# Gated scan and ELU feed-forward: activation and ring rows a little more than a row apart, and the first product read and written backwards

## What is computed

```
sig = 1.0 / (1.0 + np.exp(-f_logit))
f = lower_bound + (1.0 - lower_bound) * sig
for t in range(S):                      # 6080 steps
    h = f[:, t] * h + (1.0 - f[:, t]) * x[:, t]
    y[:, t] = h
h = y.reshape(12160, 256) @ w_in        # 256 -> 2048
g = np.where(h > 0.0, h, np.exp(np.minimum(h, 0.0)) - 1.0)
out = g @ w_out                         # 2048 -> 256
```

## Time and profile before

| | before |
|---|---|
| median of two runs | 989.77 us (989.63 and 989.91) |
| span of the profiled execution | 987.9 us |
| PE busy | 983.2 us, 4362 matmuls |
| PE weight loads busy | 817.7 us |
| ACT, DVE, POOL busy | 791.6, 726.4, 633.2 us |
| chain that ended last | PE 100% |
| granted TensorE clock | 1.000 |

### The profile page before, as it was taken

How to read it: one execution, slowest core, us unless ns; L and a number is a source line. 1 busy time by engine, 2 the same in 40 slices (tenths; PEclk the granted TensorE clock), 3 DMA queues, 4 the chain that set the end, 5 groups by cost and what they waited for, 6 DMA issues and landing times.

```text
span 987.9 us, 15016 instructions
## 1 busy us (share of the span) xinstructions
PE 983.2 (100%) x4362; PEld 817.7 (83%) x4362; DVE 726.4 (74%) x916; ACT 791.6 (80%) x1424; POOL 633.2 (64%) x477
## 2 busy tenths in 40 slices
PE   9999999999999999999999999999999999999998
PEld 6998888888888888888888888888888888888887
DVE  6987876976886796697688679678768867956444
ACT  7988878878888887877887887888788788787775
POOL 2588796576567558557656756856765765675444
PEclk9999999999999999999999999999999999999999
DMA  7212012002102201200210210120021021001001
GB/s 265 66 33 91 0 35 63 33 1 76 54 1 60 69 1 42 64 21 10 65 53 0 64 63 0 51 66 10 25 61 42 0 74 53 0 0 45 1 1 43
DMA packets 23078, 42.02 MB, mean 43 GB/s; under 512 B 2560, under 2 KB 4096, under 8 KB 23040
## 3 DMA queue, kind: packets, MB, share of 16 engines
q1 hardware_dynamic: 22752, 41.10, 12.9%
q10 hardware_dynamic: 288, 0.46, 0.1%
HBM read 29.10 MB, written 12.45 MB: 42 GB/s over the span
## 4 chain that ended last, share of the span: by engine, by line
PE 100%; DVE 0%; POOL 0%; issue 0%; POOLq 0%
PE acc L886 17%; PE acc L888 17%; PE acc L887 17%; PE h L859 14%; PE h L855 14%; PE h L857 14%; PE h L992 1%; PE h L993 1%; PE h L991 1%; PE h L999 1%; PE h L958 0%; PE h L968 0%; PE acc L991 0%; PE acc L992 0%; PE acc L993 0%; PE acc L958 0%
## 5 line engine op out<-in xcount | busy, mean ns | idle before, releaser
L327 POOL TENSOR_TENSOR g_lo<-e,g_hi 128x512 fp32r<-128x512 f32 (+1 forms) x384 | 519.4, 1363 | 348.6 <-ACT g_hi L471 347.7
L457 ACT ACTIVATE e<-h 128x512 f32<-128x512 f32 (+1 forms) x379 | 225.6, 595 | 151.7 <-PE h L859 129.2
L710 DVE SCALAR_TENSOR_TENSOR e<-e,h 128x512 f32<-128x512 f32 (+1 forms) x379 | 256.3, 676 | 70.7 <-ACT e L463 70.4
L887 PE MATMUL acc<-g_lo,w_out_hi 128*128 128x512 f32 (+1 forms) x768 | 297.2, 387 | 0.0
L886 PE MATMUL acc<-g_hi,w_out_hi 128*128 128x512 f32 (+1 forms) x768 | 297.2, 387 | 0.0
L888 PE MATMUL acc<-g_hi,w_out_lo 128*128 128x512 f32 (+1 forms) x768 | 297.2, 387 | 0.0
L463 ACT ACTIVATE e<-e 128x512 f32<-128x512 f32 (+1 forms) x384 | 241.5, 629 | 9.6 <-issue 1.2
L471 ACT CAST g_hi<-e 128x512 fp32r<-128x512 f32 (+1 forms) x384 | 232.4, 605 | 16.9 <-DVE e L710 16.9
L859 PE MATMUL h<-a_hi,w_in_lo 128*128 128x512 f32 x616 | 239.7, 389 | 0.0
L855 PE MATMUL h<-a_hi,w_in_hi 128*128 128x512 f32 x616 | 239.7, 389 | 0.0
L857 PE MATMUL h<-a_lo,w_in_hi 128*128 128x512 f32 x616 | 239.6, 389 | 0.0
(11 more groups left out here) (77 smaller groups left out, 563.0 us busy)
## 6 DMA issues: line engine op xcount, KB each, us to landing
opening<-forget_logit SPq DMA_DIRECT2D x44, 256.0 KB, 2.6
x<-value SPq DMA_DIRECT2D x44, 256.0 KB, 2.7
out<-out_sb SPq DMA_DIRECT2D x44, 256.0 KB, 2.0
w_in_raw<-w_in SPq DMA_DIRECT2D x8, 256.0 KB, 6.1
w_out_raw<-w_out SPq DMA_DIRECT2D x8, 256.0 KB, 6.8
out<-out_sb SPq DMA_DIRECT2D x4, 224.0 KB, 1.9
x<-value SPq DMA_DIRECT2D x3, 224.0 KB, 6.6
opening<-forget_logit SPq DMA_DIRECT2D x2, 224.0 KB, 6.6
```

The lines of the kernel that those rows point to most:

```text
L327: nc.gpsimd.tensor_tensor(g_lo[:, t % RING, 0:w], e[:, t % TILES, 0:w], g_hi[:, t % RING, 0:w].bitcast(F32), ALU.subtract).then_inc(g_lo_r ...
L457: nc.scalar.activation(e[:, i, 0:w], bank_of(j, t)[:, 0:w], ACT.Relu, scale=-1.0).then_inc(r_ready, 1)
L710: nc.vector.scalar_tensor_tensor(e[:, t % TILES, 0:w], e[:, t % TILES, 0:w], -1.0, bank_of(j, t)[:, 0:w], ALU.add, ALU.max).then_inc(g_rea ...
L887: nc.tensor.matmul(bank, hi, g_lo[:, t % RING, 0:w], start=False, stop=False)
```

## The change

It has three parts.

1. Rows of `a_hi` and `a_lo` are 516 elements apart in the place of 512 (`STEP_A`, 16 bytes), and rows of the rings `g_hi` and `g_lo` 520 (`STEP_G`, 32 bytes). Only 512 of them are used.
2. `carry`, `slope` and `offset` are placed ahead of the weights, `room_before` and `room_of_edge` go, and `room_of_a_hi` and `room_of_g_hi` put the starts of `a_hi` and `g_hi` a multiple of 512 bytes behind the start of the weights. `w_plain_lo4` to `w_plain_lo7`, which are used in block 0 alone, are laid into unused rows, rounded down to 32 bytes.
3. In `product` (blocks 1 to 11) the moving row is read, and the PSUM bank written, from the last column to the first. Each column's result lands where it did. `second`, `first_products` and `first_product` read forwards as before.

What part 1 and 2 make of the starts, in bytes past a multiple of 512, counted from the start of the weights, where every weight tile is at 0 in both kernels:

| moving row | before | after |
|---|---|---|
| `a_hi`, set `par`, row `k` | 0 | 16 (6 par + k), 0 to 176 |
| `a_lo`, set `par`, row `k` | 0 | 192 + 16 (6 par + k), 192 to 368 |
| `a4_hi`, `a4_lo` | 0 | 384 |
| `g_hi`, slot `s` | 0 | 32 s, 0 to 224 |
| `g_lo`, slot `s` | 0 | 256 + 32 s, 256 to 480 |

No instruction moves on any engine, none is added and none is removed; waits are the same too.

```diff
+STEP_A = 4
+STEP_G = 8
...
-        sb("room_before", [P, -base % 512], mybir.dt.uint8)
+        carry = sb("carry", [P, BATCH, HALVES, 1])
+        slope = sb("slope", [P, HALVES])
+        offset = sb("offset", [P, HALVES])
         weights_at = -(-nc.sbuf_base // 32) * 32
...
-        sb("room_of_edge", [P, P - EDGE])
...
-        a_hi_at = -(-nc.sbuf_base // 32) * 32
-        a_hi = sb("a_hi", [P, 2, PRODUCTS - 1, TILE], F32R)
+        a_hi_at = weights_at + -(-(nc.sbuf_base - weights_at) // 512) * 512
+        sb("room_of_a_hi", [P, a_hi_at - nc.sbuf_base], mybir.dt.uint8)
+        a_hi = sb("a_hi", [P, 2, PRODUCTS - 1, TILE + STEP_A], F32R)
         a_lo_at = -(-nc.sbuf_base // 32) * 32
-        a_lo = sb("a_lo", [P, 2, PRODUCTS - 1, TILE], F32R)
...
+        a_lo = sb("a_lo", [P, 2, PRODUCTS - 1, TILE + STEP_A], F32R)
...
-        g_hi = sb("g_hi", [P, RING, TILE], F32R)
-        g_lo = sb("g_lo", [P, RING, TILE], F32R)
...
+        g_hi_at = weights_at + -(-(nc.sbuf_base - weights_at) // 512) * 512
+        sb("room_of_g_hi", [P, g_hi_at - nc.sbuf_base], mybir.dt.uint8)
+        g_hi = sb("g_hi", [P, RING, TILE + STEP_G], F32R)
+        g_lo = sb("g_lo", [P, RING, TILE + STEP_G], F32R)
...
-            return a_hi[:, par, k], a_lo[:, par, k]
+            return a_hi[:, par, k, 0:TILE], a_lo[:, par, k, 0:TILE]
...
-                nc.tensor.matmul(bank[:, 0:w], hi, a_h[:, 0:w], start=start, stop=False,
-                                 skip_group_check=True)
...
+                back, a_h, a_l = bank[:, 0:w][:, ::-1], a_h[:, 0:w][:, ::-1], a_l[:, 0:w][:, ::-1]
+                nc.tensor.matmul(back, hi, a_h, start=start, stop=False, skip_group_check=True)
+                nc.tensor.matmul(back, hi, a_l, start=False, stop=False, skip_group_check=True)
+                return nc.tensor.matmul(back, lo, a_h, start=False, stop=True, skip_group_check=True)
```

More of the change, by code:

```diff
@@ L107, in gated_scan_elu_ffn @@
         x = sb("x", [P, BATCH, HALVES, TILE])
-        a_hi_at = -(-nc.sbuf_base // 32) * 32
-        a_hi = sb("a_hi", [P, 2, PRODUCTS - 1, TILE], F32R)
+        a_hi_at = weights_at + -(-(nc.sbuf_base - weights_at) // 512) * 512
+        sb("room_of_a_hi", [P, a_hi_at - nc.sbuf_base], mybir.dt.uint8)
+        a_hi = sb("a_hi", [P, 2, PRODUCTS - 1, TILE + STEP_A], F32R)
         a_lo_at = -(-nc.sbuf_base // 32) * 32
-        a_lo = sb("a_lo", [P, 2, PRODUCTS - 1, TILE], F32R)
-        for p, at in ((4, a_lo_at + 4 * TILE * P3), (5, a_lo_at + 4 * TILE * P6),
-                      (6, a_lo_at + 4 * TILE * P7), (7, a_hi_at + 4 * TILE * P3)):
-            w_plain_low.append(nc.alloc_sbuf_tensor_at(f"w_plain_lo{p}", [P, 4, P], F32R, offset=at))
+        a_lo = sb("a_lo", [P, 2, PRODUCTS - 1, TILE + STEP_A], F32R)
+        place = 4 * (TILE + STEP_A)
+        for p, at in ((4, a_lo_at + place * P3), (5, a_lo_at + place * P6),
+                      (6, a_lo_at + place * P7), (7, a_hi_at + place * P3)):
+            w_plain_low.append(nc.alloc_sbuf_tensor_at(f"w_plain_lo{p}", [P, 4, P], F32R, offset=at // 32 * 32))
         a4_hi = sb("a4_hi", [P, TILE], F32R)
@@ L118, in gated_scan_elu_ffn @@
         p5 = sb("p5", [P, TILE])
-        g_hi = sb("g_hi", [P, RING, TILE], F32R)
-        g_lo = sb("g_lo", [P, RING, TILE], F32R)
-        carry = sb("carry", [P, BATCH, HALVES, 1])
-        slope = sb("slope", [P, HALVES])
-        offset = sb("offset", [P, HALVES])
+        g_hi_at = weights_at + -(-(nc.sbuf_base - weights_at) // 512) * 512
+        sb("room_of_g_hi", [P, g_hi_at - nc.sbuf_base], mybir.dt.uint8)
+        g_hi = sb("g_hi", [P, RING, TILE + STEP_G], F32R)
+        g_lo = sb("g_lo", [P, RING, TILE + STEP_G], F32R)
         h = ctx.enter_context(nc.psum_tensor("h", [P, 4, TILE], F32))
```

## The result

The changed kernel takes 1013.69 us (two runs, 1013.68 and 1013.70) against 989.77 us: slower by the ratio 1.0242, 95% interval 1.0212 to 1.0271. Forecast were 968.5 us and a range of 947 to 1013 us.

A forecast was written before the change was run, and what follows sets the result against it. PE never waits, so time was taken as matmul count times interval, 226.7 ns. 987.9 - 19.4 - 1.8 = 966.7 us; the runs' median lies 1.9 us above, 968.6, given as 968.5 us; range 947 to 1013 us.

The forecast's parts named there:

- What bounds the kernel: Whole kernel: PE waits for nobody, so time is the count of matmuls times their interval, 226.7 ns.
- That the addresses count: Matmuls of blocks 1 to 11: row and weight reads get in each other's way by address; up to 9.7 ns each.
- rival B: Both products: addresses don't count, the 13.4 ns over streaming belong to the form; 989.8 us, chance 0.20.
- I take half of the gain: Row steps of 16 and 32 bytes, both products: half of 9.7 ns goes, 4.9 ns less a matmul.
- A: Rival, blocks 1 to 11: part of the interval's excess goes, the forecast itself; 968.5 us, chance 0.50.
- I take the same half gain: Backwards reading in `product`, 1848 matmuls: half the gain; with the row steps 3960 x 4.9 = 19.4 us less.
- Block 0: Block 0 and the opening, 448-column matmuls on shifted rows: the same proportion of gain, 368 x 4.9 = 1.8 us less.
- The other engines: Writing the shifted rows on ACT, POOL and DVE: costs nothing, hidden by the ring of eight rows.
- C: Rival, both products: the steady pattern is lost, 4.1 ns more a matmul, 16 us more; 1006 us, chance 0.24.
- rows 8: Earlier trace where block 0 and block 1 matmuls mix: same instructions 230.8 ns apart on average, one 0.24 us, against 226.7.
- D: Rival, `product`: writing a bank backwards costs PE its rate, 394 us more; 1384 us, chance 0.06.
- The check that I had put down: PE timeline after, steady stretch: each product's intervals tell the rivals apart; idle time or products moving oppositely disprove the prediction.

The follow-up runs named there:

- e4: Kernel before with 64 bytes of room ahead of `a_hi`, so all moving rows begin 64 bytes past their weight tile's multiple of 512, all forwards: 997.9 us, ratio 1.0082.
- e5: Kernel before with 128 bytes of room ahead of `a_hi`, all rows read forwards: 1012.6 us, ratio 1.0230.
- the groups: Kernel before with groups of 24 more matmuls at its end, each with another start, direction, length or type; start 0 with 512 columns forwards settled at 226.65 ns.
- `p2_starts`: Kernel before with 33 groups of 24 matmuls at its end (other starts, shifted weight tiles, one-sided backwards, other lengths, bf16); start 288 settled at 233.4 ns.
- e2: Changed kernel with the first product read forwards again, row steps and placing kept: 1010.5 us, ratio 1.0209 against the kernel before.
- e1: Kernel before with only the backwards reading and writing in the first product, all starts unchanged: 1007.5 us, ratio 1.0179.
- e7: Kernel before with only the PSUM bank written backwards in the first product, rows read forwards: 989.6 us, ratio 0.9999.

## Why the prediction was wrong

**What bounds the kernel: right.** The time is PE's count of matmuls times their interval; before, after and in all variants the idle time ahead of PE's groups of both products in blocks 1 to 11 is 0.0.

**That the addresses count: right, but the earlier trace rows didn't show it.** The addresses there are all equal. What it shows is a stream out of its even pattern behind a change of length, as rival B said; that the starts of the rows count too was a guess, which e4, e5 and the groups bear out. The groups show the way back to the even pattern in the open: in `p2_starts` the group of start 0 that follows start 288 has the intervals 230, 236, 228, 233, 231 and then 226.65 on the average, while the one that follows a group in the even pattern has it from the first.

**The step that failed is the sign of the row steps: "I take half of the gain".** It took the bf16 interval for what float32r would have without conflict. It isn't. float32r has 13.3 ns over its streaming at 256, 320, 384 and 512 columns alike, with row and weight tile at the same start, and no one of the 64 groups with 512 columns settled under 226.65 ns. The kernel before stood at that floor already; the even pattern that I named as the argument against A is the best of all that were measured. With no gain to be had, every new start could only be equal or worse, and of 16 starts two are equal (0 and 240). The term was -4.9 ns; the runs show +5.3 for the second product, and with the steps alone (e2) +5.6 for the second and +4.8 for the first.

Whether the table explains that number can be worked out. The ring's slots stand at 0, 32, ... 224 and the low rows at 256 more, which is the same. The mean of the eight values is (226.65 + 233.2 + 228.7 + 233.5 + 233.6 + 234.1 + 233.2 + 233.5) / 8 = 232.06 ns. Measured were 231.96 in the changed kernel and 232.24 in e2. For the first product of e2, with its rows 16 bytes apart, weighed by how often each is read, the table gives 231.9 ns, measured 231.45.

It holds slot by slot too, from the recorded starts of the second product behind 98 us, though a slot's row is read only six times before the next one's turn comes:

| ring slot | 0 | 1 | 2 | 3 | 4 | 5 | 6 | 7 |
|---|---|---|---|---|---|---|---|---|
| table, ns | 226.65 | 233.2 | 228.7 | 233.5 | 233.6 | 234.1 | 233.2 | 233.5 |
| e2, ns | 228.3 | 232.7 | 230.1 | 233.0 | 233.6 | 233.9 | 232.9 | 233.4 |
| changed, ns | 230.1 | 232.9 | 228.5 | 233.2 | 232.6 | 233.1 | 232.1 | 233.1 |

**The step on backwards reading failed too: "I take the same half gain".** No run shows such a gain, and the outcome is the opposite: backwards costs 6.7 ns at nearly every start. The term was -4.9 ns. The first product, with steps and direction together, shows +6.79 ns; the direction alone is +7.15 ns in e1, and on top of the steps +2.0 ns (e2 to the changed kernel). The groups give 233.35 ns, and 236.6 at three starts, `a4_hi` and `a4_lo` at 384 among them, which makes 234.0 weighed by how often each is read. The kernel shows 233.46, and 233.8 for the product that reads `a4_hi` and `a4_lo`: the 236.6 of a long group doesn't carry over to three matmuls.

**Block 0: size small, sign wrong.** -1.8 us was set down, +0.2 us came. The table of the change has every weight tile at 0; those of `w_plain_lo4` to `w_plain_lo7`, which lie in the shifted rows, are not all there in the changed kernel, so block 0 isn't a clean test of one start.

**The other engines: right.** Rows 16 or 32 bytes on cost them nothing: ACT L475 605 ns for 605, POOL L331 1356 for 1363. They merely wait longer, ACT for PE (150.4 us for 129.2 before) and POOL for ACT (374.2 for 347.7):

```profile
L331 POOL TENSOR_TENSOR g_lo<-e,g_hi 128x512 fp32r<-128x512 f32 (+1 forms) x384 | 516.8, 1356 | 374.5 <-ACT g_hi L475 374.2
L461 ACT ACTIVATE e<-h 128x512 f32<-128x512 f32 (+1 forms) x379 | 225.0, 594 | 173.3 <-PE h L862 150.4
```

**The rivals.** C, the steady pattern is lost, is what happened. Its price of 4.1 ns and 1006 us was too low by a third; the means are 5.3 and 6.8 ns, and the 1013.69 us lie just above the range's end of 1013. A part of the shortfall is the timeline's rounding: by the recorded starts the twelve intervals of the earlier trace rows are 228 to 236 ns, 231.6 on the average, so 4.9 ns and some 1009 us could have been read, and the 0.24 us are 236 ns. The rest is that rows 8 is another disturbance, a change of length at equal starts.

B is half right. That addresses don't count is refuted by e4 and e5. That the 13.4 ns belong to the form is borne out as far as the runs go: 13.3 ns stay at the best start. The rule of the Trainium skill that went with B ("SBUF — State Buffer", "Who interferes with whom": two independent read ports, PE never waits on anyone) leaves no room for what was measured here: a shift of the weight tile alone by 32 bytes takes 226.65 to 233.4 ns.

D is refuted by e7. The Trainium skill's rule on patterns in PSUM ("Advanced Engine Details and Errata", "PSUM Cachelines") doesn't reach a step of minus one: 226.65 ns. The 215.7 ns for 512 columns of the Trainium skill ("TensorE: Matmul & The Clock Gate", "Wait — 56ns, not 53.3ns?") agree with bf16 at 215.9, not with float32r at 226.65.

**The check that I had put down worked.** Intervals that change from slot to slot with period eight and a mean above 226.7 were named for C, and that is what the means by slot above show; the two products moved the same way, so nothing cancelled.

**What stays open.** What the 13.3 ns of float32r are: no start, width of the tile or length of the row that was tried goes below them. How the row's read and the weight load hinder each other isn't shown either, only argued from the starts: the runs show that the difference of the starts counts, with a period of 256 bytes (but for 240 and 496: 226.65 and 233.3 ns), that the direction of the read counts, and that row and tile shifted together by 16 or 48 bytes don't follow the difference alone. Why a shorter weight load makes the interval longer isn't known. No group ran without a weight load beside each matmul. The weight tiles were never read in the other direction, so whether it is the direction itself that costs or its relation to that of the weight load stays open.

A kernel that beats both wasn't found. The one gain in sight is in block 0: 448 columns at the starts 64 and 160 settle at 200 ns for 202.7, at most 368 x 2.7 = 1.0 us or 0.1%. In e4, where block 0's rows stand at 64, it came to 0.7 us; block 0 at such a start with the other blocks at 0 wasn't tried.

## What to carry to other kernels

Where PE is never idle, read its interval and ask first whether it is at the floor of its own form: compare with the same form at other lengths, not with another type. In float32r with a weight load for each matmul, let rows and weight tiles of 512-column matmuls begin at the same place of 256 bytes, at a multiple of 32, and read forwards; steps of 16 and 32 bytes from row to row cost 2% here. A timeline with two decimals is too coarse for such differences over a few matmuls. Before a layout is changed in a full kernel, some groups of 24 matmuls behind its last one give the interval of each layout in one run, and they foretold the kernels to 0.1% for 64 bytes (with two small errors that cancelled) and to 0.5% for 128.

## What the runs showed of the hardware

- The interval of a float32r matmul of 512 columns at 2.4 GHz is 226.65 to 236.7 ns, by the start of its row against its weight tile (period 256 bytes, but for 240 and 496) and the direction of the read; bf16 is 215.9 ns at four starts and backwards.
- At start 0 it has some 13.3 ns over its streaming time at 256, 320, 384 and 512 columns, 16 to 20 at 448, 16.7 at 480 and 58 at 128.
- A shorter weight load (32 columns, 109 ns for 188) doesn't shorten the interval: 231.8 ns for 226.65.
- Writing a PSUM bank backwards is free (226.65 ns); reading a row backwards costs 6.7 ns.
- A disturbed stream needs one to nine matmuls of 512 columns to find the even pattern again; with five (start 0 behind start 288) that is 25 ns in all, and in e1 it took the unchanged second product from 226.67 to 228.72 ns.
